# A spectral mix and two feed-forward layers: the second matmul of each layer as seven block products, and the two layers one after the other

## The reference

```python
def _attn_ref(x, filt_r, filt_i) -> np.ndarray:
    X = np.fft.rfft(x, axis=1)
    F = (filt_r + 1j * filt_i)[None, :, :]
    Y = X * F
    y = np.fft.irfft(Y, n=x.shape[1], axis=1)
    return y.astype(np.float32)
...
def _moe_ref(x, w_in, w_out, alpha) -> np.ndarray:
    h = x @ w_in
    g = np.maximum(h, 0.0) + alpha * np.minimum(h, 0.0)
    return (g @ w_out).astype(np.float32)
...
def _moe2_ref(x, w_in, w_out) -> np.ndarray:
    h = np.maximum(x @ w_in, 0.0)
    return (h * h @ w_out).astype(np.float32)
```

## Time and profile before

| | us |
|---|---|
| median of 3 runs (lowest, highest) | 1207.66 (1207.07, 1208.46) |
| time of the profiled execution | 1208.74 |
| span of the profiled execution, first to last instruction | 1207.0 |
| TensorE busy in the span | 1181.6 |
| VectorE, ScalarE, GpSimd busy | 787.5, 522.3, 134.0 |

### The profile page before, as it was taken

The page is one execution under the profiler, slowest core; times in us unless marked ns, Lnnn a source line. Parts: engine busy times, 40 slices in busy tenths (PEclk is TensorE's granted clock), DMA queues, the critical chain, the costliest instruction groups (busy, mean ns, idle before and its releaser), DMA issues.

```text
span 1207.0 us, 17786 instructions
## 1 busy us (share of the span) xinstructions
PE 1181.6 (98%) x6683; PEld 1139.8 (94%) x6683; DVE 787.5 (65%) x1475; ACT 522.3 (43%) x1041; POOL 134.0 (11%) x104
## 2 busy tenths in 40 slices
PE   7889999999999999999999999999999999999998
PEld 3578999999999999999999999999999999999998
DVE  0748855587766876677655775567655775567654
ACT  4734554533555335542344224532344224532354
POOL 0536611111211111110000000000000000000000
PEclk9989999999999999999999999999999999999999
DMA  8993121222022122110000100010000100000000
GB/s 243 256 312 111 32 55 46 80 55 57 27 74 79 27 61 58 50 48 1 1 2 13 39 2 1 14 40 1 1 1 14 39 1 1 13 14 1 1 4 24
DMA packets 48054, 57.25 MB, mean 47 GB/s; under 512 B 4192, under 2 KB 39136, under 8 KB 46944
## 3 DMA queue, kind: packets, MB, share of 16 engines
q1 hardware_dynamic: 47968, 56.11, 16.5%
HBM read 37.35 MB, written 18.74 MB: 46 GB/s over the span
## 4 chain that ended last, share of the span: by engine, by line
PE 88%; DVE 6%; DMA 2%; ACT 2%; issue 1%; SPq 0%; POOL 0%; ACTq 0%; DVEq 0%
PE bank L881 14%; PE bank L886 14%; PE bank L882 14%; PE bank L901 14%; PE bank L896 13%; PE bank L897 13%; PE bank L862 2%; DVE g L757 2%; DVE g_lo L733 2%; PE bank L799 1%; DVE g L746 1%; DMA t_rows<-a_out_b 1%; ACT g L611 1%; DVE y_im_b L697 1%; DMA v_rows<-v_out_b 1%
## 5 line engine op out<-in xcount | busy, mean ns | idle before, releaser
L504 ACT ACTIVATE g_hi<-g 128x376 fp32r<-128x376 f32 x512 | 265.2, 518 | 546.4 <-DVE g L752 365.9
L733 DVE TENSOR_TENSOR g_lo<-g,g_hi 128x376 fp32r<-128x376 f32 x512 | 301.5, 589 | 131.3 <-ACT g_hi L504 126.8
L881 PE MATMUL bank<-in_hi,w_hi 128*128 128x376 f32 x1024 | 346.6, 338 | 3.6 <-DVE g L757 3.6
L896 PE MATMUL bank<-g_hi,w_hi 128*128 128x376 f32 x1024 | 342.4, 334 | 0.0
L882 PE MATMUL bank<-in_hi,w_lo 128*128 128x376 f32 x1024 | 342.3, 334 | 0.0
L897 PE MATMUL bank<-g_hi,w_lo 128*128 128x376 f32 x1024 | 342.0, 334 | 0.0
L901 PE MATMUL bank<-g_lo,w_hi 128*128 128x376 f32 x1024 | 258.8, 334 | 3.2 <-DVE g_lo L733 3.2
L886 PE MATMUL bank<-in_lo,w_hi 128*128 128x376 f32 x1024 | 259.5, 334 | 0.0
L746 DVE TENSOR_SCALAR g<-bank,alpha_sb 128x376 f32<-128x376 f32 x256 | 155.7, 608 | 120.5 <-PE bank L886 72.7
L757 DVE TENSOR_TENSOR g<-g 128x376 f32<-128x376 f32 x256 | 159.2, 622 | 108.4 <-ACT g L611 108.2
L881 PEld LDWEIGHTS bank<-in_hi,w_hi 128*128 128x128 f32 x1024 | 192.7, 188 | 9.9 <-DVE g L757 7.0
(11 more groups left out here) (51 smaller groups left out, 486.5 us busy)
## 6 DMA issues: line engine op xcount, KB each, us to landing
filt_b<-filt SPq DMA_DIRECT2D x36, 256.0 KB, 4.3
w_raw<-w SPq DMA_DIRECT2D x8, 1024.0 KB, 11.7
t_raw_b<-t_rows SPq DMA_DIRECT2D x24, 256.0 KB, 3.9
v_rows<-v_out_b SPq DMA_DIRECT2D x24, 256.0 KB, 2.5
vc<-v_rows SPq DMA_DIRECT2D x32, 192.0 KB, 3.9
out<-out_sb SPq DMA_DIRECT2D x32, 188.0 KB, 1.9
x_raw_b<-x SPq DMA_DIRECT2D x8, 384.0 KB, 7.8
t_rows<-a_out_b SPq DMA_DIRECT2D x16, 192.0 KB, 4.0
```

The lines of the kernel that those rows point to most:

```text
L504: return act.activation(dst, src, ACT.Copy)
L733: dve.tensor_tensor(g_lo[:, s % GR, :], g[:, s % 2, :], g_hi[:, s % GR, :], ALU.subtract).then_inc(g_lo_ready, 1)
L881: pe.matmul(o, w_in(w_h, k, f), x_h[:, slot, k, :], start=(k == 0), stop=False)
L896: pe.matmul(o, w_out(w_h, half, f), g_hi[:, s % GR, :], start=(f == 0), stop=False)
```

## The change

**Seven products.** The down matmul of a layer is G (tokens x 2048) by W (2048 x 256). Two hidden tiles (a pair, p) and the two halves of W make a 2x2 block of W; two token halves of a group and the same two hidden tiles make a 2x2 block of G. In place of eight block products the kernel does the seven of Winograd's form of Strassen's method: sums of blocks of G (T1N, T2, T3, T4) and of W (S1N to S4) are formed first, seven products are accumulated in `m_ps` over the 8 pairs, and `combine` makes the four results of them at the end of a group.

**Groups and slots.** Tokens go in 12 groups of 500 or 504 (two halves of 250 or 252). A slot n is one pair of one group in one layer, 8 slots to a group, 96 to a layer, 192 in all. TensorE does in slot n `up(n)` (12 matmuls of 500 or 504 columns) and `down(n - 2)` (21 of 250 or 252). Per slot VectorE finishes the activation (two instructions), makes T1N and T3 in one, and the lo part of all seven pieces in one; GpSimd makes T2 and T4; ScalarE does two relus and one hi copy of seven pieces.

**Layers in sequence.** All groups pass layer 1 and are stored to `z_rows`, then all pass layer 2 (loaded to `zin`). Only one layer's weights are on the core: those of layer 2 are summed, split and stored by tiles in slots 48 to 86, and loaded over layer 1's from slot 90 on. Layer 1's weight sums and lo parts for pairs 2 to 7 are made by VectorE in slots 0 to 5.

**Spectral work of batch 1.** The units of transform A stand in slots 4 to 15, one or two a slot. Unit u of the other twelve starts in slot B(u) = 18 + 2u.

The core of the diff, added lines:

```diff
+HALF = (252, 250, 250, 252, 250, 250) * BATCH
...
+SLOTS_1 = GROUPS * FP
+LAG = 2
+RING = 3
...
+PRODUCTS = ((0, 0, A11, B11), (1, 0, A12, B21), (1, 1, S2, T2), (2, 0, S1N, T1N),
+            (2, 1, S3, T3), (3, 0, S4, B22), (3, 1, A22, T4))
...
+A_COUNT = {4: 1, 6: 1, 7: 1, 8: 2, 9: 2, 10: 2, 11: 2, 12: 2, 14: 2, 15: 1}
+A_SLOT = [s for s, n in A_COUNT.items() for _ in range(n)]
+B_SLOT = [18 + 2 * u for u in range(B_UNITS)]
+VC_P, Y_P, IN_P = 3, 5, 6
+EARLY_W = 2
+W2_SLOT = [48 + 5 * q for q in range(FP)]
```

GpSimd, then ScalarE, a slot each:

```diff
+                    for u in range(A_UNITS):
+                        if A_SLOT[u] == n:
+                            pool.wait_ge(f1.x_hi_ready, done(u))
+                            low(f1.x_lo[:, u % 2, :], f1.x_raw[:, u % f1.xs, :], f1.x_hi[:, u % 2, :], f1.x_lo_ready)
+                    for u in range(B_UNITS):
+                        if B_SLOT[u] + 2 == n:
+                            pool.wait_ge(f1.y_hi_ready, done(u))
+                            low(f1.y_lo[:, :], f1.y_re[:, 0, :], f1.y_hi[:, :], f1.y_lo_ready)
+                        if B_SLOT[u] == n:
+                            t_low(f1, u, 0, 0)
...
+                pool.wait_ge(t13_ready, n + 1)
+                pool.tensor_tensor(g_raw[:, r, T2, 0:h], g_raw[:, r, B22, 0:h], g_raw[:, r, T1N, 0:h],
+                                   ALU.add).then_inc(t2_ready, 1)
+                pool.wait_ge(t2_ready, n + 1)
+                pool.tensor_tensor(g_raw[:, r, T4, 0:h], g_raw[:, r, B21, 0:h], g_raw[:, r, T2, 0:h],
+                                   ALU.subtract).then_inc(t4_ready, 1)
+                if n < SLOTS_1:
+                    for u in range(B_UNITS):
+                        if B_SLOT[u] + 1 == n:
+                            add(f1, u, 0)
...
+                for j in range(2):
+                    act.wait_ge(h_done, 2 * n + j + 1)
+                    if j == 0 and n >= RING:
+                        act.wait_ge(down_done, n - RING + 1)
+                    act.activation(g_raw[:, r, 2 * j:2 * j + 2, 0:h],
+                                   h_ps[j][:, 0:2 * h].rearrange("p (j d) -> p j d", j=2), ACT.Relu,
+                                   scale=-1.0 if n < SLOTS_1 else 1.0).then_inc(relu_ready, 1)
...
+                    for u in range(A_UNITS):
+                        if A_SLOT[u] + 1 == n:
+                            a_copy(f1, u, u // f1.outs, u % f1.outs, u % 2, u % f1.outs)
+                    for u in range(B_UNITS):
+                        if B_SLOT[u] + 1 == n:
+                            for c in range(2):
+                                swap(u, c)
...
+                        if A_SLOT[u] == n:
...
+                            copy(f1.x_hi[:, u % 2, :], f1.x_raw[:, u % f1.xs, :]).then_inc(f1.x_hi_ready, 1)
+                    for u in range(B_UNITS):
+                        if B_SLOT[u] == n:
+                            t_high(f1, u, u, 0, 0)
+                if n > 0:
+                    q = (n - 1) % RING
+                    hq = HALF[(n - 1) // FP % GROUPS]
+                    act.wait_ge(t4_ready, n)
+                    copy(g_hi[:, q, :, 0:hq], g_raw[:, q, B11:T4 + 1, 0:hq]).then_inc(g_hi_ready, 1)
...
+                if p == LAG - 1 and g > 0:
...
+                    copy(ct[:, M1, 0:hc], m_ps[0][:, 0:hc]).then_inc(m1_ready, 1)
...
+                    for u in range(B_UNITS):
+                        if B_SLOT[u] + 1 == n:
+                            y_high(u)
+                if n + EARLY_W < FP:
+                    w_high(n + EARLY_W)
```

VectorE: weight sums, combine, and the rest of a slot behind the activation:

```diff
+                dve.scalar_tensor_tensor(out=raw[:, S1N, :], in0=raw[:, A21, :], scalar=-1.0, in1=raw[:, A22, :],
+                                         op0=ALU.mult, op1=ALU.subtract).then_inc(signal[1], 1)
+                dve.wait_ge(signal[1], 3 * at + 1)
+                dve.scalar_tensor_tensor(out=raw[:, S2, :], in0=raw[:, S1N, :], scalar=-1.0, in1=raw[:, A11, :],
+                                         op0=ALU.mult, op1=ALU.subtract).then_inc(signal[1], 1)
+                dve.tensor_tensor(raw[:, S3, :], raw[:, A11, :], raw[:, A21, :], ALU.subtract).then_inc(signal[1], 1)
+                dve.wait_ge(signal[1], 3 * at + 3)
+                dve.tensor_tensor(raw[:, S4, :], raw[:, A12, :], raw[:, S2, :], ALU.subtract).then_inc(signal[0], 1)
...
+            def w_low(p):
+                dve.wait_ge(w_hi_ready, p + 1)
+                dve.tensor_tensor(w_lo[:, p, :, :], w_raw[:, p, :, :], w_hi[:, p, :, :],
+                                  ALU.subtract).then_inc(w_lo_ready, 1)
...
+                dve.tensor_tensor(ct[:, C11:U2 + 1, 0:h], two(1), ct[:, M1:M1 + 1, 0:h].to_broadcast([P, 2, h]),
...
+                dve.tensor_tensor(ct[:, U4:U3 + 1, 0:h], two(2), ct[:, U2:U2 + 1, 0:h].to_broadcast([P, 2, h]),
...
+                dve.tensor_tensor(ct[:, C22, 0:h], m_ps[2][:, 0:h], ct[:, U3, 0:h], ALU.add).then_inc(c_ready, 1)
+                dve.wait_ge(down_done, (g + 1) * FP)
+                dve.tensor_tensor(ct[:, C12:C21 + 1:C21 - C12, 0:h], two(3), ct[:, U4:U3 + 1, 0:h],
+                                  ALU.add).then_inc(c_ready, 1)
...
+                    if j == 0 and p == IN_P and g + 1 < 2 * GROUPS:
+                        in_low(g + 1)
+                dve.wait_ge(g_ready, 2 * n + 2)
+                dve.tensor_tensor(g_raw[:, r, T1N:T3 + 1, 0:h], g_raw[:, r, B11:B22 + 1, 0:h],
+                                  g_raw[:, r, B12:B12 + 1, 0:h].to_broadcast([P, 2, h]),
+                                  ALU.subtract).then_inc(t13_ready, 1)
+                if p == LAG - 1 and g > 0:
+                    combine(g - 1)
+                if n > 0:
+                    g_low(n - 1)
+                if n < SLOTS_1:
+                    for u in range(B_UNITS):
+                        if B_SLOT[u] + 1 == n:
+                            product_re(f1, u, 0, 0, 0)
+                            product_im(f1, u, u % B_HALF, 0, 0, 0)
+                if n + EARLY_W < FP:
+                    w_sums(n + EARLY_W)
+                    w_low(n + EARLY_W)
```

TensorE: the waits of `up` and `down`, the products, and the order of a slot (`y_group` is `y_chunk` for a group of 6 pairs of tokens):

```diff
+                if g == 0:
+                    pe.wait_ge(w_lo_ready, p + 1)
...
+                for j in range(2):
+                    if n > 0:
+                        pe.wait_ge(g_ready, 2 * n + j - 1)
...
+                pe.wait_ge(g_hi_ready, n + 1)
+                for b, side, tile, piece in PRODUCTS:
+                    o = m_ps[b][:, side * 256:side * 256 + h]
...
+                    pe.matmul(o, w_hi[:, p, tile, :], g_hi[:, q, piece - B11, 0:h],
...
+                pe.wait_ge(g_lo_ready, n + 1)
+                for b, side, tile, piece in PRODUCTS:
...
+                    mm = pe.matmul(o, w_hi[:, p, tile, :], g_lo[:, q, piece, 0:h], start=False, stop=last,
...
+            for n in range(2 * SLOTS_1):
+                g, p = divmod(n, FP)
+                up(n)
+                if n >= LAG:
+                    down(n - LAG)
+                if n < SLOTS_1:
+                    if p == Y_P and g + 1 < GROUPS:
+                        pe.wait_ge(in_lo_ready, (g + 1) * KD)
+                        pe.wait_ge(f1.a_out_ready, done(sum(s < n for s in A_SLOT) - 1))
+                        pe.wait_ge(f1.im_ready, done(sum(s < n for s in B_SLOT) - 1))
+                        pe.wait_ge(f1.v_ready, done(sum(s + 2 < n for s in B_SLOT) - 1))
+                        y_group(g + 1)
...
+                    for u in range(A_UNITS):
+                        if A_SLOT[u] == n:
...
+                            transform_a(f1, u, u % 2)
+                    for u in range(B_UNITS):
+                        if B_SLOT[u] + 2 == n:
...
+                            inverse(f1, u, 0, 0)
+                    for u in range(B_UNITS):
+                        if B_SLOT[u] == n:
+                            pe.wait_ge(in_lo_ready, (ys + 1) * KD)
...
+                            spectrum(f1, u, 0, 0)
```

731 lines of the change are left out of this document (340 added, 391 removed).

## The result

| | before | after |
|---|---|---|
| median, us (lowest, highest) | 1208.06 (1207.07, 1211.67) | 1273.18 (1271.5, 1274.63) |
| span of the profiled execution | 1207.0 | 1269.6 |
| mean granted clock of the span | 0.996 | 0.959 |

The ratio is 1.0533, 95% interval [1.0507, 1.0559]: 65 us slower, where 33 were forecast. The direction and the mechanism held, and the time lies in the whole range of 1205 to 1280, but not in the likeliest part of it, 1225 to 1255; the loss was forecast at half its size.

What follows compares the result with a forecast made beforehand. TensorE's matmuls were taken to set the time: its own sum 1139, plus waits 9, 19, 13 and 52 and slow clock 8, gave 1240 of span, 1241 us. Likeliest 1225 to 1255 (0.55), whole range 1205 to 1280.

Steps and rivals of the forecast that it cites:

- TensorE's work: Layer matmuls: `up` 529.0 and `down` 462.9 us, together 991.9 against 1058.0 before, 66 saved; a slot 5.17.
- The rival of narrow matmuls at 0.111: `down` matmuls at 0.111 us, not 0.1148: 12 less, 1229, with smaller losses down to 1206; chance 0.10.
- VectorE and GpSimd exclude each other: An exclusive lock held for the whole instruction; T2 and T4 compete with `g_low` in every slot, hidden in an ordinary one.
- Slots 0 to 5: VectorE needs 8.1 us a slot against 5.17, for weight sums, `w_hi` waits and subtracts; `up` waits for `w_lo`: 19 us.
- Transform A: Slots 4 to 15: TensorE waits for GpSimd's `x_lo`, 1.6 us in each of six two-unit slots; 13 us in all.
- The twelve units: Slots 18 to 42: the chain to the next `up` takes 15.35 us a pair against 11.7; 52 us of waits.
- The long gaps are in the six slots just named: I add 8: Slow clock after long idle stretches, charged only in slots 21, 25, 29, 33, 37 and 41: 8 us.
- about 0.6 more each: In slots 21, 29 and 37 `y_group` waits for the `y_im`, about 0.6 us more each.
- ScalarE's relu late behind `y_hi`: Sign in slots 18 to 42: next slot's relus stand behind `y_high` on ScalarE, at 10.4 us after `up`.
- The rest of layer 1: 469 to 700 us: loss forecast at 2.3 us.
- TensorE stays fed: Rival: chains overlap, pairs of slots from 18 under 11.7 us, 1160 us; chance 0.12, another 0.03 for a loss cut to two thirds.
- rival 2: Dearer narrow matmuls, GpSimd's short ones near 1.29, or slow clock in every gap: 1255 to 1280; chance 0.17, 0.03 beyond.

Runs made afterwards that it cites:

- x_best: Kernel after with x_order's, x_relufirst's, x_wsum's moves, `t_lo` before `y_lo`, `spectrum` before `inverse`, earlier `x_hi`, `x_lo`, `t_hi`, `t_lo`, `inverse` a slot later: 1226.24 us.
- x_wsum: Kernel after, with VectorE doing the four weight sums of slots 0 to 5 ahead of the previous slot's `g_low`: 1264.13 us.
- x_warm: Kernel after, with throwaway matmuls: 7 ahead of each unit's inverse, 18 ahead of `y_group` in the twelve units' slots: 1258.02 us.
- x_nob: Kernel after without batch 1's twelve later units; batch 1's tokens come from batch 0's rows: 1179.01 us.
- x_relufirst: Kernel after, with ScalarE doing a unit's `y_high` behind the next slot's relus and `t_high`, not ahead of them: 1277.71 us.
- x_yg: x_best with the next group's `y_group` issued between `up` and `down` of slot 8k+6, `in_hi` and `in_lo` behind that slot's relus and differences: 1209.63 us.
- x_gfirst: x_yg with batch 1's inverse as one full-precision matmul, and the layer's own steps ahead of the spectral ones on ScalarE, VectorE and GpSimd: 1201.57 us.
- x_order: Kernel after, with VectorE doing the filter products (`y_re`, `y_im`) ahead of `combine` and `g_low`: 1241.69 us.

## Why the prediction was right, and where it was short

**TensorE's work: right.** The first `up` came at 79.31 (forecast 79.3). Matmuls of 252 columns start 0.116 apart and of 504 0.228; a slot is 5.18 to 5.20 (5.17). T2 and T4 take 0.73 when nothing blocks them (0.73 forecast, between 0.63 and 1.29). The rival of narrow matmuls at 0.111 is out. The Trainium skill (TensorE: Matmul & The Clock Gate, Back-to-back issue gap) states its gap rule for a single matmul by itself; by it 250 columns would be 0.107, and the trace of this stream shows 0.115. The turn from layer 1 to layer 2 costs nothing, as forecast: slots 88 to 103 take 5.21 each.

**VectorE and GpSimd exclude each other: right, and still under-used.** After, GpSimd's T2 beside VectorE's `g_low`, two timelines of that kernel:

```profile
268.05 1.97 DVE L775 TENSOR_TENSOR g_lo<-g_raw,g_hi 128x1750 fp32r<-128x1750 f32 x1
```

```profile
268.20 2.40 POOL L493 TENSOR_TENSOR g_raw<-g_raw 128x250 f32<-128x250 f32 x1 [0.62 <-DVE g_raw L797]
```

T2, 0.73 alone, ends 0.58 after the record of `g_low`: nearly all of its run lies behind it. The trace agrees with the exclusive lock of the Trainium skill (SBUF — State Buffer, Who interferes with whom). The forecast used this for T2 and T4 and was right there. My own expectation for x_best left it out for `y_im`.

**Slots 0 to 5: right chain, 5 short.** The wait for `w_hi` is the 1.44 named, and x_wsum took it away. But a slot took VectorE 9.07, not 8.1, five times over. That is 5 of the 8 us by which the table's first row is short; the other 3 are open. The term that was mis-sized is the sums of weights, "four of 128 columns at 0.29 to 0.35". In slot 1 two of them met GpSimd's T2 and T4; timeline of VectorE and then of GpSimd:

```profile
94.78 0.82 DVE L701 SCALAR_TENSOR_TENSOR w_raw<-w_raw 128x128 f32<-128x128 f32 x1
95.63 0.77 DVE L704 SCALAR_TENSOR_TENSOR w_raw<-w_raw 128x128 f32<-128x128 f32 x1
```

```profile
95.53 0.72 POOL L496 TENSOR_TENSOR g_raw<-g_raw 128x252 f32<-128x252 f32 x1
```

The four take 2.1 us there, not 1.2. The exclusion was charged to T2 and T4 and not to the sums.

**Transform A: right in sum.** Slots 8 to 15 lose 11.7 us, of the 13 forecast for slots 4 to 15. The clock, 0.93 from 130 to 200 us, is part of them and was not charged, so the waits by themselves were charged too high.

**The twelve units: right mechanism, short by 14.** The step that failed is "The long gaps are in the six slots just named: I add 8". The clock fell after every unit's wait, also where the longest was 1.8 us, at `y_hi`, and not in six slots. x_warm shows what it costs there at least: 15 us, 0.3 to 0.9 in a plain pair, 1.5 with `combine`, 2.1 with `y_group`; with the 4.8 of its own matmuls that fill no gap it is some 20, where 8 were charged. The second part is "about 0.6 more each" for `y_group`: `up`, `down`, `inverse`, `spectrum` and the next `up` all stand behind it, so the pair is 7.6 + 2.8 + 2.76 + 2.4 + 1.4 + 2.76 = 19.7 at full clock by the forecast's own prices, not 18.75; x_warm, less its own 1.6, shows 19.5. The two parts make some 15 of the 17 us by which the twelve units exceed their 60 in x_nob. The forecast's 43, 8 and three times 0.6 also add up to 53, not 52.

"ScalarE's relu late behind `y_hi`" was named as a sign, and it is in the rows. x_relufirst shows that taking `y_high` out of its way wins nothing, since `y_hi` itself is waited for.

**The rest of layer 1: 9 us not foreseen.** Groups there take 46.1 to 46.5 us with 44.1 of TensorE's work, in layer 2 41.6 with 41.4. What differs is the sums and low parts of layer 2's weights, which I priced at nothing. In x_nob, where nothing is woven in from slot 16 on, the groups without them can be told from those with them. Windows of that kernel, each from one `y_group` to the next, slots 30 to 37 and 54 to 61:

```profile
287.76:332.04 44.28, 44.17 (x291) 40.24 (x290) 37.23 (x38) 23.79 (x28) 21.74 (x17) 1.00 0.11 26
422.44:468.69 46.25, 44.62 (x290) 40.53 (x289) 41.48 (x47) 25.31 (x29) 23.69 (x16) 1.00 0.26 83
```

The 2 us a group appear with layer 2's weights. In the kernel after, their sums and low parts stand behind `g_low` on VectorE:

```profile
529.17 1.99 DVE L775 TENSOR_TENSOR g_lo<-g_raw,g_hi 128x1764 fp32r<-128x1764 f32 x1
531.08 2.16 DVE L819 TENSOR_TENSOR s_lo<-s_raw,s_hi 128x1408 fp32r<-128x1408 f32 x1
533.16 1.37 DVE L790 SCALAR_TENSOR_TENSOR g_raw<-g_raw,rest_sb,bank 128x500 f32<-128x500 f32 x2
```

VectorE is without a pause here. That it is VectorE's part, and not ScalarE's copies or the loads of these weights, was argued from the rows and not tried.

**The rivals.** "TensorE stays fed" (1160) was wrong for the code as written. Its mark, under 11.7 us a pair, is not met by any change of order alone: the best of those, x_yg, has 13.4. Pairs of 11.9 exist in x_gfirst, with the plain inverse, which also takes two steps out of the chain. Of rival 2's three causes two are out, dearer narrow matmuls and slow short instructions on GpSimd. "The slow clock in every gap" is seen in the traces. That 1273 lies in its 1255 to 1280 is in part luck: of the 32 us above 1241 the clock in the units makes some 12, and 9 come from layer 2's weights and 5 from the sums of layer 1's, which no rival named.

## What to carry to other kernels

When a change makes the fast engine faster, its slack in a woven-in chain goes first: price each chain end to end, in queue order, with all that is issued behind its waiting instruction. Then charge the clock for every gap that the chain opens on TensorE, not only for the longest. A step on one of two engines that exclude each other is priced with what the other does at that time, also if it is short. An order that pays while a chain is tight (x_order, 31 us) need not pay once it is loose (x_gfirst), so try it again after each change of the slots.

## What was not expected of the hardware

- Behind a unit whose longest single wait was 1.8 us TensorE's matmuls ran at the 1.2 GHz level (0.42 for 504 columns) for 2.5 to 3 us more; matmuls whose results are thrown away, in the gap, took 15 us off the kernel.
- The four `y_im`, 1.13 us in all when alone, take 2.8 to 3.3 when GpSimd runs `t_lo`, T2 and T4 in the same time. There VectorE's short instructions are the ones held up; beside one long `g_lo` it was GpSimd's, 2.91 in place of 1.26.
- A full-precision matmul of 512 columns in one instruction, about 0.85, stood in for three rounded ones, 0.70, and two instructions on other engines, at no loss in time.
